# Moving GpSimd's sums of the second weight and VectorE's splits of weights and tokens to other groups of a fused attention and mixture-of-experts kernel

## What is computed

```python
def _moe_ref(x, w_gate, w1, w2):            # N, D, E, F = 1536, 512, 8, 1024
    logits = x @ w_gate
    logits = logits - logits.max()
    P = np.exp(logits)
    for _ in range(8):                       # rows and columns are balanced in turn
        P /= P.sum(1, keepdims=True) + 1e-09
        P /= P.sum(0, keepdims=True) + 1e-09
        P *= N / E
    out = np.zeros((N, D))
    for e in range(E):
        h = np.maximum(x @ w1[e], 0.0)
        out += P[:, e:e + 1] * (h @ w2[e])
    return out
```

## Time and profile before

| | |
|---|---|
| time, median of 3 runs | 1378.83 us (1375.6 to 1379.8) |
| the profiled execution's own time | 1377.87 us |
| its span in the trace | 1376.0 us |
| PE busy | 1300.2 us (94%) |
| DVE, ACT, POOL busy | 946.0, 761.7 and 691.1 us |
| TensorE's mean granted clock | 0.986 |

### The profile page before, as it was taken

One profiled execution on the slowest core, in us unless ns is written; L12 is line 12 of the kernel. 1 busy time (PEld: TensorE's weight loads), 2 busy tenths in 40 slices (PEclk: granted clock), 3 DMA queues, 4 the chain that ended last, 5 costly groups with the idle time before them and its releaser, 6 DMA issues.

```text
span 1376.0 us, 31280 instructions
## 1 busy us (share of the span) xinstructions
PE 1300.2 (94%) x12075; PEld 1017.1 (74%) x12075; DVE 946.0 (69%) x1540; ACT 761.7 (55%) x1429; POOL 691.1 (50%) x859
## 2 busy tenths in 40 slices
PE   7999999989989999999999999999999989998997
PEld 3767667865478887787888788788888867556675
DVE  6999999645766666676666667666656554567984
ACT  6999999653244544554455445545434555225762
POOL 4666787604446566567656656666545410021211
PEclk9999999999999999999999999999999999999999
DMA  7555441012344341333434133322400032367950
GB/s 176 134 118 122 111 99 43 2 53 68 115 165 138 101 146 51 128 92 131 139 100 147 51 124 88 125 85 85 154 1 17 24 98 102 128 209 283 323 205 20
DMA packets 128740, 154.83 MB, mean 113 GB/s; under 512 B 9296, under 2 KB 88696, under 8 KB 128608
## 3 DMA queue, kind: packets, MB, share of 16 engines
q1 hardware_dynamic: 126144, 149.63, 35.4%
q0 software_dynamic: 2240, 3.35, 0.7%
q10 hardware_dynamic: 224, 0.02, 0.0%
HBM read 115.59 MB, written 39.36 MB: 113 GB/s over the span
## 4 chain that ended last, share of the span: by engine, by line
PE 65%; POOL 12%; DVE 8%; ACT 7%; issue 4%; DMA 2%; SPq 0%; ACTq 0%; POOLq 0%; DVEq 0%
PE ps L2127 7%; PE ps L2128 7%; PE ps L2129 7%; PE ps L2044 5%; PE ps L2048 5%; PE ps L2047 5%; PE ps L1969 5%; PE ps L2068 5%; PE ps L2070 5%; PE ps L2069 5%; PE ps L1957 2%; POOL parts L867 2%; PE ps L1959 2%; POOL parts L862 2%; PE ps L1941 2%
## 5 line engine op out<-in xcount | busy, mean ns | idle before, releaser
L2068 PE MATMUL ps<-x,w 128*128 128x256 f16 x1344 | 369.8, 275 | 42.6 <-ACT parts L1099 26.5
L2070 PE MATMUL ps<-x,w 128*128 128x256 f16 x1344 | 370.1, 275 | 0.0
L2069 PE MATMUL ps<-x,w 128*128 128x256 f16 x1344 | 369.7, 275 | 0.0
L2127 PE MATMUL ps<-w_seven,h_ring 128*128 128x256 f16 x1008 | 277.0, 275 | 5.4 <-DVE h_ring L1555 4.8
L2128 PE MATMUL ps<-w_seven,h_ring 128*128 128x256 f16 x1008 | 276.7, 275 | 0.0
L2129 PE MATMUL ps<-w_seven,h_ring 128*128 128x256 f16 x1008 | 276.5, 274 | 0.0
L2068 PEld LDWEIGHTS ps<-x,w 128*128 128x128 f16 x1344 | 132.1, 98 | 78.8 <-ACT parts L1099 30.4
L862 POOL TENSOR_TENSOR parts<-parts 128x256 f32<-128x256 f32 x72 | 63.5, 882 | 164.6 <-ACT parts L1115 164.6
L2070 PEld LDWEIGHTS ps<-x,w 128*128 128x128 f16 x1344 | 132.6, 99 | 16.4
L2069 PEld LDWEIGHTS ps<-x,w 128*128 128x128 f16 x1344 | 132.5, 99 | 15.0
L2127 PEld LDWEIGHTS ps<-w_seven,h_ring 128*128 128x128 f16 x1008 | 99.6, 99 | 22.4 <-DVE h_ring L1555 8.5
(11 more groups left out here) (265 smaller groups left out, 3257.8 us busy)
## 6 DMA issues: line engine op xcount, KB each, us to landing
w_ready<-w_out SPq DMA_DIRECT2D x48, 448.0 KB, 4.6
w_seven<-w_ready SPq DMA_DIRECT2D x42, 512.0 KB, 5.0
w_parts<-w1a SPq DMA_DIRECT2D x128, 128.0 KB, 2.7
w_parts<-w2a SPq DMA_DIRECT2D x48, 256.0 KB, 2.9
w_in<-w1b SPq DMA_DIRECT2D x4, 2048.0 KB, 8.7
w_in<-w2b SPq DMA_DIRECT2D x4, 2048.0 KB, 9.4
w_in_b<-w1b SPq DMA_DIRECT2D x4, 2048.0 KB, 10.8
w_in_b<-w2b SPq DMA_DIRECT2D x4, 2048.0 KB, 9.7
```

Of the source, the lines that this page charges most:

```text
L2068: pe.matmul(acc, w_hi, x_hi, start=(opens and kt == 0), stop=False, skip_group_check=not opens)
L2069: pe.matmul(acc, w_hi, x_lo, start=False, stop=False, skip_group_check=not opens)
L2070: last = pe.matmul(acc, w_lo, x_hi, start=False, stop=(kt == 1), skip_group_check=not opens)
L2127: pe.matmul(acc[:, p, :], a_hi, b_hi, start=begins, stop=False, skip_group_check=True)
```

## The change

1. `sum_w2` of piece 2 (in an expert's first batch) and of piece 0 of the expert after it (in the third) moves on GpSimd from behind the batch's second group (`place == 1`) to behind its fourth (`place == FQ - 1`). These are ten calls of four operations, five of each kind.
2. In expert 0, VectorE splits the last pair of tokens (pair 5) in group 6 and no longer in group 5, the gates in group 7 and no longer in 5, and each of the four parts of w2 one group later (groups 7 to 10; before, 6 to 9). ScalarE still makes their high parts in groups 6 to 9.
3. In expert 7, the low part of each part of w2 is made in the next group, behind that group's `h_low`, and not straight behind L1574 of its own.

```diff
+X_SPLIT_AT = {1: 2, 2: 3, 4: 4, 6: 5}
 FIRST_W2_AT = {6: 0, 7: 1, 8: 2, 9: 3}
 LAST_W2_AT = {NGROUPS - GE + 2 + c: c for c in range(4)}
...
-                elif place == 1 and batch == 0 and seven:
+                elif place == FQ - 1 and batch == 0 and seven:
                     sum_w2(ahead, 2)
-                elif place == 1 and batch == 2 and ahead + 1 < E - 1:
+                elif place == FQ - 1 and batch == 2 and ahead + 1 < E - 1:
                     sum_w2(ahead + 1, 0)
...
-            def first_expert_step(g):
-
-                if g in (1, 2, 4, 5):
-                    split_x({1: 2, 2: 3, 4: 4, 5: 5}[g])
-                if g == 5:
+            def expert_step(g):
+
+                if g - 1 in LAST_W2_AT:
+                    plain_w2_part(E - 1, LAST_W2_AT[g - 1])
+                if g >= GE:
+                    return
+                if g in X_SPLIT_AT:
+                    split_x(X_SPLIT_AT[g])
+                if g == LOGITS_AT:
                     split_gates()
...
-                if g in FIRST_W2_AT:
-                    plain_w2_part(0, FIRST_W2_AT[g])
+                if g - 1 in FIRST_W2_AT:
+                    plain_w2_part(0, FIRST_W2_AT[g - 1])
...
-                    group(k, ready, lambda: first_expert_step(k) if k < GE else None)
+                    group(k, ready, lambda: expert_step(k))
...
-                    if k in LAST_W2_AT:
-                        plain_w2_part(E - 1, LAST_W2_AT[k])
```

## The result

The changed kernel takes 1338.37 us (median of 4 runs, 1335.08 to 1339.98) where the kernel before takes 1379.32: ratio 0.9708, 95% interval 0.9687 to 0.9729. The forecast was 1341. The profiled execution took 1335.08 us, its span is 1333.3 us against 1376.0, so the two traces differ by 42.7 us.

A forecast was written before the change was run, and what follows sets the result against it. TensorE's waits for ScalarE and VectorE, and the half-clock stretches behind some, were taken to bound the kernel. Parts of 24.2, 8.0 and 4.3 us sum to 36.5, from 1377.87 to 1341 us; range 1332 to 1355.

The forecast's parts named there:

- Gross 31.0: Experts 1 to 6: 23.2 us of waits and 10.2 us of half speed go, 2.4 us of L1555 waits come back.
- Product 7, 0.25 each: In sevens with a piece, TensorE waits for VectorE's sums slowed beside GpSimd: ten times, 2.5 us lost.
- The second batches, 0.85 each: GpSimd's next sum starts 2.4 us later, so VectorE's L1570 comes late in five second batches: 4.3 us lost.
- product 4: In the seven, ScalarE waits up to 2.4 us for the piece, but L1192 is done 1.2 us before product 4.
- Part 2: Expert 0: L1570's waits of 6.8 us and one half-speed stretch go; 8.0 us gained, bounds 6 and 8.8.
- Part 3: Expert 7: ScalarE's wait for L1551 shortens by 1.1 us four times; 4.3 us gained, bounds 2 and 5.
- No new waits: Rival 1: delays in the sevens find room and parts 2 and 3 reach upper bounds; 44.8 us gained, 1333; chance 0.15.
- VectorE gives way twice: Rival 2: L1558 and L1560 each wait a whole 0.72 us GpSimd operation; 7 us lost at product 7, 1346; chance 0.10.
- Second batches that stall for good: Rival 3: L1492, L1579, L1570 get over 2 us late, half speed follows; 14.5 us more, 1356; chance 0.10.
- half speed does not go with the waits: Rival 4: TensorE's half-speed stretches are only loosely tied to the waits; 12 us stay, 1353; chance 0.07.
- Little moves: Rival 5: L1099 also waits for `h_lo`, so only a third of part 1 comes; 1357; chance 0.05.
- a piece that isn't loaded: Rival 6: in the seven GpSimd waits 6.6 us for w2's transfer; 71 us more, 1412, slower; chance 0.03.

The follow-up runs named there:

- nearly empty: The changed kernel with the ten moved pieces summing one of 256 columns, so the output is wrong: 1334.23 us, ratio 0.9683 to the kernel before.
- part 1 alone: The kernel before with only the ten GpSimd pieces moved behind the fourth group: 1349.38 us, ratio 0.9793.
- the split moved: The changed kernel with VectorE's split of the seven's second piece put behind the next batch's first group: 1335.72 us, ratio 0.9691 to the kernel before.
- part 2 alone: The kernel before with only VectorE's splits of plain weights and tokens in expert 0 made later: 1372.52 us, ratio 0.9957.
- the waiting piece: The changed kernel with GpSimd waiting for VectorE's low sums before it begins the piece: 1341.80 us, ratio 0.9735 to the kernel before.
- one group earlier: The changed kernel with the ten pieces behind the batch's third group: 1369.22 us, ratio 0.9943 to the kernel before.
- one sum later: The changed kernel with the ten pieces behind the seven's own sum: 1368.96 us, ratio 0.9934 to the kernel before.
- part 3 alone: The kernel before with only VectorE's low parts of w2 in expert 7 made one group later: 1374.00 us, ratio 0.9975.
- the two halves: The kernel before with only the first batches' five pieces moved (1363.53 us), or only the third batches' five (1362.09 us).

## Why the prediction was right

**The mechanism** was right in all three parts. The waits for L1099 and L1570 were the price, and each part alone took its own of them away and left the others. In all I forecast 36.5 us, and 41 came by the medians, 42.7 by the two traces: the forecast time was 2.6 us too high, within its range, and it was short mostly in part 1.

**Part 1** gave 29.6 us (the stretch, 622.7 to 593.1) where I said 24.2. Its terms:

- Gross 31.0 was right as a sum, but by luck: two errors cancel. Half speed costs 0.7 to 1.1 us a time and not 1.7 less 0.4: six of them about 5, not 7.8. But a removed wait gives more than its length in the list: 2.32 us for one of 2.19, after the 0.2 paid at product 7, so 2.5; ten are worth 25 to 26 and not 23.2. Most of the difference is in how the list counts: from the end of a matmul of 0.27 us, although the next one would have started 0.11 us behind its start. That makes 0.16 us more for each wait, 2.35 for the 2.19 at 807.24 us before.
- Before also had a wait of 1.0 us for L1120 at 514.71 us, worth 1.3 us in that batch. After has none, but a kernel with the pieces moved and nearly empty has one of 1.04 us in the same batch, and part 1 alone one of 0.7, so the gain isn't shown to be the change's.
- Product 7, 0.25 each: measured 0.20, and 0 where the contention is taken away. Ten times, 2.0 us for 2.5. The due time that I read from the trace was exact.
- **The second batches, 0.85 each, were the step that was mis-sized.** They cost 0 to 0.2 us each, and 0.3 us in sum (the stretch with the split moved, 592.8 against 593.1), for 4.3. I added up a delay of 2.4 us for GpSimd's next sum. Its piece took 4.32 us there and not the 5.0 that I allowed, and the copy ended at the very moment it was due. The reserve was as thin as I said: 0.86 us more and it costs 0.75.
- ScalarE's L1077 waits 1.67 us (I allowed 2.4), and product 4 had 2.5 us to spare (I said 1.2).

**Part 2** was forecast at 8.0 and measured at 8.0 by the traces, alone and in the whole; by the medians part 2 alone gave 5.2, uncertain by 2. **Part 3** was forecast at 4.3 and gave 5.1 to 5.3: beside the 3.2 us of waits for L1099 the waits for L1136 fell from 1.7 to 1.1 us, and one of 0.5 for L1199 went, which I had not counted; the 0.16 us that the list leaves out of each wait make up most of the rest.

**The rivals.** No new waits (1333) is nearest in size, yet the waits are there, 0.2 us at product 7. That VectorE gives way twice is out in its price; its mechanism is not (below). Second batches that stall for good would need more than 0.86 us of further delay: with that much, the waiting piece, they wait at most 1.2 us and no half speed follows. That half speed does not go with the waits is out for after, although the tie is loose. Little moves is out by the size of part 1, and a piece that isn't loaded by GpSimd's timeline, where L844 follows the sum's last operation without a wait (437.09).

## What to carry to other kernels

A piece of side work on a shared engine costs what comes due next behind it, so look for the place between two due times and count both chains: here one group earlier and one sum later cost 31 us each. A wait of TensorE in the list is worth somewhat more than its length (0.16 us here), because the list counts from the end of a matmul that the next one would have overlapped, and a stretch at half speed somewhat less than the half of it, because it hides the next small waits. Waits of 0.1 to 0.2 us are in no list: look for gaps between starts.

## What the runs showed of the hardware that I had not expected

**VectorE and GpSimd take turns by whole instructions.** I had argued against that from two operations that lost 0.92 us where two of GpSimd's would be 1.4. The starts and ends in the seven of after say that the turns are exact: L844 ends at 437.81 and L1559 at 438.36, L846 at 438.95, L1561 at 440.04, L849 at 440.61. Each ends 0.55 to 0.59 us (GpSimd) or 0.55 and 1.09 us (VectorE) behind the other's end, a little less than it takes alone (0.72; 0.69 and 1.23), as if its start-up of some 0.14 us went on beside. The loser loses only what is left of the other's instruction. In the nearly empty piece GpSimd's two operations of one column last until VectorE's end (L846 to 438.04, L1559 to 437.99; L852 to 439.30, L1561 to 439.26): 0.67 and 1.04 us for work of 0.18. The Trainium skill (SBUF — State Buffer, the glossary on the shared port pair) says that the pair is held for the full instruction and that the loser fully blocks, and the trace agrees. What was wrong is the second rival's price for it, a whole operation of 0.72 us each time: the two lost 0.51 and 0.41 us.

**Of two equal waits one has half speed behind it and the other not.** Of the ten like waits of 2.2 to 2.9 us before, six have a 3.4 us stretch at the lower clock behind them; of the same ten (2.2 to 3.2 us) with part 2 alone seven, with part 3 alone five; of five and five in the two halves, three and two; of ten of 2.89 us behind the third group, four. None of the waits of 1.2 and 1.4 us in the kernel with the piece behind the seven's sum has one. It is not the kind of batch that decides, and the traces speak against plain chance: within a trace the stretches start on one beat, and what goes with them is where the wait lies against it. With the third batches' pieces moved, the wait from 441.21 to 443.40 us lies between two beats and has a stretch from 444.3 on. The equally long one from 794.81 to 797.00 us is cut near its middle by a beat (795.9, counted on from 444.3) and has none. Of the 55 waits of over 2.1 us between 260 and 1000 us in the seven traces that have such waits, 28 have one, and ordered by where they lie the two kinds do not mix. No run moved a wait against the beat on purpose, so this is read off and not tested.
